# Moving the first unit's scale and split a few steps earlier in the attention loop

## The reference, cut to what matters

```python
scores = scale * np.matmul(q, k.transpose(0, 1, 3, 2))
scores = cap * np.tanh(scores / cap)
attn = np.exp(scores - np.max(scores, axis=-1, keepdims=True))
attn = attn / (np.sum(attn, axis=-1, keepdims=True) + 1e-09)
x = heads_side_by_side(np.matmul(attn, v))          # [1792, 768]
h = x @ w_in; r = np.maximum(h, 0.0); y = (r * r) @ w_out
logits = y @ w_gate                                 # picks 224 rows for each of 8 experts
out[mask] = np.maximum(y[mask] @ w1[e], 0.0) @ w2[e]
```

## Time and profile before

| | us |
|---|---|
| median of 3 runs | 1089.48 (1088.46 to 1089.95) |
| profiled execution, its own time | 1089.84 |
| its span, from the first to the last instruction | 1088.1 |
| attention's last product with v ends, `up` begins | 315.87 after the span's start |

### The profile page before, as it was taken

How to read it: one execution, slowest core, us unless ns; L and a number is a source line. 1 busy time by engine, 2 the same in 40 slices (tenths; PEclk the granted TensorE clock), 3 DMA queues, 4 the chain that set the end, 5 groups by cost and what they waited for, 6 DMA issues and landing times.

```text
span 1088.1 us, 24810 instructions
## 1 busy us (share of the span) xinstructions
PE 1044.1 (96%) x9468; PEld 846.3 (78%) x9468; DVE 826.6 (76%) x1685; ACT 601.6 (55%) x950; POOL 199.5 (18%) x319
## 2 busy tenths in 40 slices
PE   6999999999989999999999999999995999999996
PEld 3444444444469899999999999999995989888885
DVE  5999998999967666665685666556658999999971
ACT  5887777998936233333452110111516688777881
POOL 2544443444330000000000000000002122212201
PEclk9999998999999999999999999999996999999998
DMA  4751211112033000000330000003246566677401
GB/s 104 189 146 53 66 51 51 51 51 59 18 129 114 2 2 1 2 1 1 109 126 27 27 2 27 27 27 143 96 164 216 194 240 250 257 282 269 166 14 51
DMA packets 56996, 103.53 MB, mean 95 GB/s; under 512 B 6224, under 2 KB 34640, under 8 KB 56912
## 3 DMA queue, kind: packets, MB, share of 16 engines
q1 hardware_dynamic: 54352, 91.33, 25.0%
q0 software_dynamic: 2560, 11.01, 3.3%
HBM read 91.32 MB, written 11.01 MB: 94 GB/s over the span
## 4 chain that ended last, share of the span: by engine, by line
PE 74%; DVE 14%; issue 8%; ACT 2%; POOL 1%; DMA 1%; DVEq 0%; POOLq 0%; SPq 0%; ACTq 0%
PE psum L1543 21%; PE psum L1476 20%; PE psum L1677 10%; PE psum L1663 9%; DVE arena L972 5%; PE psum L1409 3%; PE psum L1429 2%; PE psum L1420 2%; PE psum L1592 2%; DVE arena L964 1%; DVE arena L967 1%; PE psum L1563 1%; DVE arena L952 1%; POOL arena L529 1%; PE psum L1645 1%
## 5 line engine op out<-in xcount | busy, mean ns | idle before, releaser
L1543 PE MATMUL psum<-arena 128*128 128x224 f16 x2304 | 232.3, 259 | 0.0
L1476 PE MATMUL psum<-arena 128*128 128x224 f16 x2304 | 223.7, 259 | 0.0
L1476 PEld LDWEIGHTS psum<-arena 128*128 128x128 f16 x2304 | 220.0, 98 | 2.9 <-issue 1.5
L1543 PEld LDWEIGHTS psum<-arena 128*128 128x128 f16 x2304 | 215.8, 98 | 1.0 <-issue 0.2
L529 POOL TENSOR_SCALAR arena<-arena 128x448 f32<-128x448 f32 x168 | 107.7, 652 | 166.6 <-DVE arena L954 166.5
L1429 PEld LDWEIGHTS psum<-arena 128*112 128x112 f32 x672 | 71.7, 135 | 73.2 <-POOL arena L529 38.6
L661 ACT ACTIVATE arena<-arena 128x448 f32<-128x448 f32 x168 | 125.7, 750 | 4.6 <-DVE arena L974 4.2
L1677 PE MATMUL psum<-arena 128*112 128x384 f16 x768 | 127.1, 326 | 0.4 <-issue 0.4
L1677 PEld LDWEIGHTS psum<-arena 128*112 128x112 f16 x768 | 99.3, 130 | 24.8 <-issue 0.8
L1663 PE MATMUL psum<-arena 128*128 128x224 f16 x1152 | 114.2, 262 | 3.5 <-DVE arena L1322 2.0
L1663 PEld LDWEIGHTS psum<-arena 128*128 128x128 f16 x1152 | 111.6, 99 | 5.8 <-DVE arena L1322 2.4
(11 more groups left out here) (227 smaller groups left out, 1306.1 us busy)
## 6 DMA issues: line engine op xcount, KB each, us to landing
arena<-moe_w SPq DMA_DIRECT2D x16, 3072.0 KB, 12.2
arena<-moe_w_out SPq DMA_DIRECT2D x32, 384.0 KB, 4.1
arena<-moe_w_in SPq DMA_DIRECT2D x16, 384.0 KB, 5.6
arena<-q SPq DMA_DIRECT2D x24, 224.0 KB, 2.9
arena<-k SPq DMA_DIRECT2D x24, 224.0 KB, 3.1
arena<-v SPq DMA_DIRECT2D x24, 224.0 KB, 2.6
y_rows<-arena SPq DMA_DIRECT2D x16, 336.0 KB, 3.2
arena<-y_rows,arena POOLq DMA_INDIRECT x16, 4.5
```

Source lines behind the costliest of these rows:

```text
L1476: last = pe.matmul(out, w_split[:, f, z, k * 128:(k + 1) * 128], x[u % 2][:, k, :], start=(k == 0 and m == 0), stop=(k == KD - 1 and m == 2))
L1543: last = pe.matmul(out, w_split[:, k, z, m * 128:(m + 1) * 128], g[u][:, k, :], start=(k == 0 and j == 0 and (0 < u < NU - 1 or m % 2 == 0 ...
```

## The change

`x0_step` gives other steps: stage 1 moves from step 90 to step 86, stage 2 from step 92 to step 89, stage 3 from step 94 to step 91. The matmul of stage 2 moves behind the scores of its step on TensorE. No instruction is added or removed.

```diff
         def x0_step(it, i):
 
-            return i // 2 if is_step(it, NIT - 1) and i in (2, 4, 6) else 0
+            if is_step(it, NIT - 2) and i == 6:
+                return 1
+            return {1: 2, 3: 3}.get(i, 0) if is_step(it, NIT - 1) else 0
...
+                if chunk_live(g + 3):
+                    scores()
                 if x0_step(it, i) == 2:
                     pe.wait_ge(s_xm, 1)
                     pe.matmul(x_bound, ones_f, x_max, start=True, stop=True).then_inc(s_xa, 1)
-                if chunk_live(g + 3):
-                    scores()
                 if chunk_live(g):
                     prob_T()
```

## The result

| | before | after |
|---|---|---|
| first series, 11 runs each, median, us | 1089.73 (1086.22 to 1091.07) | 1092.44 (1090.18 to 1093.16) |
| ratio, 95% interval | | 1.0027 (1.0018 to 1.0037) |
| profiled span | 1088.1 | 1090.7 |
| transposes of chunk 86 to attention's last product | 283.32 to 315.87 = 32.55 | 283.85 to 318.96 = 35.11 |

The change made the kernel 0.27% slower, some 2.9 us; I had forecast +0.98 us. By it the changed kernel is 2.56 us longer. Behind it next to nothing changed: 1090.7 - 318.96 = 771.7 us against 1088.1 - 315.87 = 772.2.

The account below looks back on a forecast made before the run. TensorE, busy for 96% of the span, was taken as the bound. Stall -1.20, x_lo +1.53, its wait +0.41 and TensorE's own order +0.24 gave +0.98 us on 1089.48, so 1090.5, range 1087.9 to 1091.9.

Parts of the forecast that it names:

- What bounds the kernel: Whole span: TensorE busy for 96%; last ten attention steps decide, VectorE has no hole there, the rest moves as a block.
- x_absmax and x_scale into full steps: Steps 86 and 89: VectorE 1.46, then 2.21 us late; TensorE's 1.0 us delay and the matmul's 0.31 go into a later gap.
- x_scale near 296.1: Sign to look for in the changed trace: the start of x_scale at its new place in step 89, in us.
- x_hi and the wait of x_lo: Step 91: x_hi starts at 301.96 on ScalarE, x_lo at about 303.40 on VectorE after a new wait of 0.41 us.
- The stall that goes: End of attention: x_lo no longer holds GpSimd's product of chunk 95; 2.33 us of stall go, 1.20 on the path.
- The drain: Last chunks: chunk 93's transposes at 306.80, chunk 95's at 310.62 instead of 309.64; end of attention +0.98 us.
- A: Rival, chance 0.14: the full steps swallow the moved work, so the drain starts earlier; -1.71 us, 1087.8.
- B: Rival, chance 0.12: x_lo holds GpSimd at its new place too, in the product of chunk 92; +1.6 us, 1091.1.
- C: Rival, chance 0.07: ScalarE becomes the bound near step 91, x_lo waits 1.8 instead of 0.4 us; +2.4 us, 1091.9.
- D: Rival, chance 0.22: x_absmax and x_scale never were the stall, only x_lo's place matters, where gain and cost cancel; 1089.5.

Follow-up runs that it names:

- experiment 1: The changed kernel with stage 3 (x_hi and x_lo) back in step 94; against the kernel before, stretch -0.94 us, ratio 0.9994.
- experiment 3: The kernel before with only stage 3 (x_hi and x_lo) moved, to step 96; against the kernel before, stretch -1.19 us, ratio 0.9990.
- experiment 5: The kernel before with one more scratch copy on ScalarE ahead of x_hi, so x_hi ends later; against before, stretch -1.20 us, ratio 0.9987.
- experiment 2: The changed kernel with 20 unused transposes filling TensorE's wait in step 93; against the kernel before, stretch +1.00 us, ratio 1.0001.
- experiment 10: The changed kernel with 8 unused transposes in TensorE's step 93; stretch 33.53 us, +0.98 us against the kernel before, one profile.
- experiment 4: All three stages in the drain, in steps 94, 96 and 97; against the kernel before, stretch -2.71 us, ratio 0.9980.
- kernel 7: As experiment 4, with the matmul of stage 2 behind its step's product with v; against the kernel before, stretch -2.88 us, ratio 0.9977.

## Why the prediction was wrong, step by step

*What bounds the kernel, and x_absmax and x_scale into full steps: right.* VectorE's rows moved by 1.46 and 0.75, and TensorE took up the 1.0 us from x_absmax before the drain. x_scale's 0.75 reaches chunk 93's transposes and leaves 0.25 at the end (experiment 1); the sum has both, inside its 306.80 and its 0.24. Among the signs, "x_scale near 296.1" doesn't follow from the working: VectorE's step 90 starts at 295.47 in the trace before, and with 1.46 that is 296.93; measured, less the 0.53 of the next paragraph, 296.91. Nothing in the sum used it.

*x_hi and the wait of x_lo: right, size included.* The changed trace stands 283.85 - 283.32 = 0.53 us later from before the first moved instruction. Taken off, the exp of chunk 93 is at 300.45 (300.46 forecast), x_hi at 301.96 (301.96) and x_lo at 303.39 (303.40). The bracket's 0.31 is counted from the recorded end of L976; counted from start to start as the forecast did, VectorE was there at 303.38 + 0.14 - 0.53 = 302.99, and the wait is 0.40 (0.41 forecast).

*The stall that goes: right.* The longest L531 is 642 ns, and experiments 3 and 5 each give 1.2 us for taking the stall alone away. What I missed is that it hung on an order of two events 0.27 us apart, so that many other edits would have removed it too, experiment 1 among them.

*The drain: right as a sum of queues, wrong as a sum of times. This is the step that failed.* It put 1.01 us for eight transposes and 0.90 for a product, from rows at full clock, behind a wait that the same working contained: chunk 92's transposes at 301.45 + 0.75 = 302.20, TensorE done with chunk 87's product 1.91 later at 304.11, and chunk 93's transposes at 306.80, 2.7 us without a matmul. The changed trace has those transposes where they were forecast (307.32 - 0.53 = 306.79), a wait of 2.61 us ahead of them and a granted clock of 0.50 behind them. From start to start the product then took 1.26 instead of 0.90, the transposes of chunk 94 1.88 instead of 1.01, the next product 1.26 instead of 0.90: 1.59 us that the sum put at nothing. Queues alone: +0.98 forecast, +1.00 and +0.98 measured with the wait filled (experiments 2 and 10). The clock: +1.56 (35.11 - 33.55). Together 2.56, which is the measured stretch. The runs' interval, 1.0018 to 1.0037 (2.0 to 4.0 us), agrees with it, and is too wide to exclude something smaller beside it.

The kernel before had a hint of it, in a place that the prediction leaves out, since the change does not touch it. TensorE's timeline before, where w_in's scale is made:

```profile
164.76 0.59 PE L1463 MATMUL psum<-arena 128*128 128x1 f32 x2 [2.26 <-DVE arena L917]
166.09 1.76 PE L1409 MATMUL psum<-arena 64*64 64x448 f32 x4 [0.74 <-DVE arena L329]
167.78 1.95 PE L1429 MATMUL psum<-arena 128*112 128x128 f32 x8
```

Waits of 2.26 and 0.74 us, and then transposes of 1.95 instead of 1.09 and scores of 1.76 instead of 0.97. That was reason enough for a fifth term, or for a rival.

*The rivals.* A fell: VectorE had no air. B fell: no product was held at the new place. C, the slower one, named the wrong engine; ScalarE was on time to 0.01 us. The forecast gave slower 0.07, and no rival was about what TensorE does after a wait. The measured 1092.44 lies above the range of 1087.9 to 1091.9, whose lower end should by A's own sum (1089.48 - 1.71) have been 1087.8. D fell in both its halves: at x_lo's new place gain and cost did not cancel, and x_absmax and x_scale matter too, since moving them as well as x_lo into the drain gains 1.52 us more (experiment 4 against 3).

*What the change should have been.* Of the places tried, the three pieces cost least not in full steps, where VectorE has no gap, but as late as the first matmul of `up` allows: kernel 7 has ratio 0.9977 (0.9968 to 0.9986) to before, which is faster than the kernel before and than the changed one (1.0027).

## What to carry to other kernels

Where three engines are full, moving work from the drain into the full steps only moves it ahead of more consumers; look for the place with slack at the far end, behind the last thing that the path needs. When a forecast puts a new wait on TensorE, go through the trace for a wait of the same length and read what the matmuls behind it took; a wait of 2.6 us here cost 1.6 us more after it was over. And before counting a contention stall as the price of an instruction's place, look how far apart the two starts are that decide who wins.

## What the runs showed of the hardware

**TensorE's clock.** In the drain it fell to half behind unbroken waits of 2.61 (twice) and 3.59 us, and not behind 1.59, 1.94 and 2.13 us, nor where 2.40 us of transposes lay in the wait (one profile each). The clock shows level by level in the rows: 1.96 for eight transposes at one and 1.08 at the other. A fall at another place also accounts for most of the difference in where the stretch starts (280.24 to 284.18). From w_in's matmul (L1463 in the kernel before) to the transposes of chunk 86 it is 115.93 us in experiment 3, 117.5 in experiments 1 and 5, and 118.5 to 118.8 in the other ten profiles. In experiment 3's profile, whose span was the shortest of all (1084.0 us), the transposes behind w_in's scale ran at full clock:

```profile
166.33 1.08 PE L1431 MATMUL psum<-arena 128*112 128x128 f32 x8
```

The waits there are the same in each kernel, 2.25 to 2.27 and 0.74 us, and 12 of the 13 profiles have a fall behind them, so a fall behind a wait near this length is not certain. In the two profiles of the changed kernel the drain had it both times. How often the drain has it in the unprofiled runs isn't shown. The mean granted clock of the whole execution points the same way, 0.9855 over the changed kernel's 11 runs and 0.9880 over the 12 of experiment 2, whose only difference is the filling; but falls at other places are in these means too.

**The port between VectorE and GpSimd.** x_lo held GpSimd's product only where x_hi was over before that product began: over 0.27 us before it in the kernel before (held), 0.4 us after it in experiments 1 and 5 (not held), although in all three x_lo itself, by its recorded start, began 0.84 to 0.88 us after the product. The simplest reading, inferred from the order in these three kernels, is that VectorE takes the SBUF ports which it shares with GpSimd once the instruction's waits are over, while the one ahead still runs. The Trainium skill (SBUF — State Buffer, "Who interferes with whom") has the order of issue decide who blocks; the trace agrees if issue is read like that, and disagrees if it is read as the recorded start. That section also has it that a VectorE instruction with at most one input in SBUF, outside its 2-port modes, does not contend with GpSimd. The trace of before agrees at another place: the row maximum L972 ran from 300.99 to 302.07 beside the two products of 300.14 to 301.39, which kept their 1.25 us. In x_lo's place it was not tried.
